# Column sums asked a product later, scaling shared by two engines, and copies and sums near the changes of pair in another order

## What is computed

```python
# attention over chunks of 32 queries, with 16 keys to the left, 8 to the right and 8 memory keys
x = attn_out.transpose(0, 2, 1, 3).reshape(3072, 512)
# first layer, d_ff = 1536
x = (x @ w_a) * (x @ w_b) @ w_out
# second layer: E = 8 experts, F = 1024, all tokens through all experts
P = exp(logits - logits.max()), logits = x @ w_gate      # 3072 x 8
for _ in range(8):
    P /= P.sum(1, keepdims=True) + 1e-09
    P /= P.sum(0, keepdims=True) + 1e-09
    P *= N / E
for e in range(E):
    h = maximum(x @ w1[e], 0)
    out += P[:, e:e+1] * (h @ w2[e])
```

## Time and profile before

| | |
|---|---|
| runs | 2672.65, 2674.56, 2677.81 us, median 2674.56 |
| profiled execution | 2671.34 us |
| its span | 2669.6 us, 39021 instructions |
| PE busy | 2586.2 us, 97% |
| DVE busy | 1570.4 us, 59% |
| ACT busy | 994.2 us, 37% |
| POOL busy | 1610.1 us, 60% |
| mean granted clock of TensorE | 0.991 of full |

### The profile page before, as it was taken

How to read it: one execution, slowest core, us unless ns; L and a number is a source line. 1 busy time by engine, 2 the same in 40 slices (tenths; PEclk the granted TensorE clock), 3 DMA queues, 4 the chain that set the end, 5 groups by cost and what they waited for, 6 DMA issues and landing times.

```text
span 2669.6 us, 39021 instructions
## 1 busy us (share of the span) xinstructions
PE 2586.2 (97%) x14946; PEld 2128.0 (80%) x14946; DVE 1570.4 (59%) x2295; ACT 994.2 (37%) x1718; POOL 1610.1 (60%) x1304
## 2 busy tenths in 40 slices
PE   7879999999999999999999999999998999999998
PEld 6658878878777888888887888888886888888887
DVE  3464454554558555555566666666667566666665
ACT  4544332232333334433333333333334433333333
POOL 0055510010276777777766777777778777777776
PEclk9999999999999999999999999999999999999999
DMA  7745644334355666666664645454544564545453
GB/s 184 162 156 210 224 178 158 143 142 159 133 208 192 254 247 226 258 256 234 234 257 183 250 183 220 182 206 188 222 180 173 188 246 173 222 182 220 184 219 115
DMA packets 193136, 530.48 MB, mean 199 GB/s; under 512 B 55544, under 2 KB 128184, under 8 KB 173752
## 3 DMA queue, kind: packets, MB, share of 16 engines
q1 hardware_dynamic: 192952, 527.99, 54.2%
HBM read 367.41 MB, written 160.60 MB: 198 GB/s over the span
## 4 chain that ended last, share of the span: by engine, by line
PE 87%; DVE 4%; POOL 3%; issue 2%; DMA 1%; ACT 1%; SPq 1%; ACTq 0%; DVEq 0%; POOLq 0%
PE bank L940 43%; PE bank L1039 21%; PE bank L1017 19%; PE bank L863 2%; POOL X L735 1%; DMA W<-w_kept 1%; POOL H L813 1%; PE bank L902 1%; DVE tmp L1595 1%; PE bank L878 1%; SPq L570 0%; PE bank L890 0%; ACT X L1260 0%; DMA Qr<-in_q_dram 0%; DVE hid L1798 0%
## 5 line engine op out<-in xcount | busy, mean ns | idle before, releaser
L940 PE MATMUL bank<-X,W 128*128 128x512 f32 x5550 | 1403.8, 391 | 22.8 <-ACT tmp L1310 9.6
L940 PEld LDWEIGHTS bank<-X,W 128*128 128x128 f32 x5550 | 1043.5, 189 | 250.9 <-issue 23.6
L813 POOL TENSOR_TENSOR H<-tmp,H 128x512 fp32r<-128x512 f32 x448 | 577.0, 1300 | 295.4 <-ACT H L1435 293.4
L1039 PE MATMUL bank<-H,W2n 128*128 128x512 f32 x2688 | 682.8, 390 | 7.7 <-DVE Y L1648 4.1
L1648 DVE TENSOR_TENSOR Y<-Y,bank 128x512 f32<-128x512 f32 x752 | 497.1, 683 | 265.1 <-PE bank L1039 265.1
L1039 PEld LDWEIGHTS bank<-H,W2n 128*128 128x128 f32 x2688 | 504.2, 188 | 115.6 <-issue 7.0
L1435 ACT ACTIVATE H<-tmp 128x512 fp32r<-128x512 f32 x448 | 276.8, 630 | 475.1 <-DVE tmp L1678 248.3
L1017 PE MATMUL bank<-W,hid 128*128 128x512 f32 x1536 | 388.1, 391 | 1.8 <-DVE Y L1625 1.8
L1017 PEld LDWEIGHTS bank<-W,hid 128*128 128x128 f32 x1536 | 289.2, 189 | 62.5 <-DVE Y L1625 2.2
L735 POOL TENSOR_TENSOR X<-Y,X 128x1024 fp32r<-128x1024 f32 x30 | 79.0, 2638 | 385.2 <-ACT X L1260 385.2
L1625 DVE SCALAR_TENSOR_TENSOR Y<-bank,gate,Y 128x512 f32<-128x512 f32 x224 | 167.0, 747 | 167.3 <-PE bank L1017 166.2
(11 more groups left out here) (111 smaller groups left out, 2160.6 us busy)
## 6 DMA issues: line engine op xcount, KB each, us to landing
W<-w_kept SPq DMA_DIRECT2D x88, 1792.0 KB, 11.1
W2n<-w2n_kept SPq DMA_DIRECT2D x64, 1536.0 KB, 8.2
w_kept<-W SPq DMA_DIRECT2D x44, 1792.0 KB, 8.1
raw<-in_moe_w_dram SPq DMA_DIRECT2D x64, 512.0 KB, 4.4
w2n_kept<-W SPq DMA_DIRECT2D x32, 1024.0 KB, 7.9
w2n_kept<-tmp SPq DMA_DIRECT2D x64, 512.0 KB, 8.0
W2n<-w2n_kept SPq DMA_DIRECT2D x64, 256.0 KB, 3.0
W<-w_kept SPq DMA_DIRECT2D x12, 1024.0 KB, 9.1
```

The costliest lines, as they stand in the source:

```text
L813: nc.gpsimd.tensor_tensor(H[:, pos, 1], hidden_at(k, pos), H[:, pos, 0].bitcast(F32), ALU.subtract).then_inc(h_lo, 1)
L940: last = nc.tensor.matmul(into[:, :], W1[:, c % 2, ws, w_slot, kc, :], X[:, pos, xs, kc, :], start=(start and kc == 0 and n == 0), stop=(k ...
L1039: last = nc.tensor.matmul(b_half[pair][half][:, :], W2n[k % 2][:, a, blk, half * P:(half + 1) * P], H[:, h, b, :], start=(q in (0, 5) and ...
```

## The change

Four things are changed.

1. `TOTALS`: the totals asked behind the products of position 6 are now asked behind those of position 0 of the next step.
2. `scale_first`: DVE scales four of the eight tiles, ACT the other four in step 5; the last scaling of the gates signals a semaphore of its own, and the accumulation into an ACT tile waits for ACT.
3. At the changes of pair: one x sum (`operand_sum 4`) moves from the end of a step into the next one, a gated product ahead of an x sum and of adds, POOL's low part of w2's sums ahead of three x pieces, a store on SP behind the loads of step 32, and the copy of x piece 6 behind copy_u.
4. On ACT, at u = 0 the pieces 2 and 3 of `up_hi` move behind copy_v; in all steps from 32 on, `hidden_hi(k, 0)` moves behind copy_v.

```diff
@@ -260,7 +260,9 @@
         g_total = sem("g_total")
         g_chain = sem("g_chain")
+        g_fin = sem("g_fin")
         g_scaled = sem("g_scaled")
+        g_scaled2 = sem("g_scaled2")
         s_out = sem("s_out")
@@ -330,6 +332,10 @@
         U_AT = (tmp[:, 4, :], tmp[:, 5, :])
         V_N, B11_T1, B12_T3, T2_AT = (tmp[:, i, :] for i in range(4))
+
+
+        def y_tile(n):
+            return Y[:, n // 2, n % 2 * TB:(n % 2 + 1) * TB]
         def hidden_at(k, pos):
@@ -646,7 +652,8 @@
                 keep_down(M1 + u)
                 keep_t_hi(u)
-                keep_t_lo(u)
+                if u + 1 < V2:
+                    keep_t_lo(u)
                 if u == 8:
                     store_gates()
@@ -655,6 +662,8 @@
                     load_gates(u)
                 fetch_blocks(u)
+                if u == V2:
+                    keep_t_lo(V2 - 1)
                 if u == V2 + 3:
                     store(0)
@@ -787,10 +796,10 @@
             block_sums(V2 - 1)
             down_lo(M1 + V2 - 1)
-            for i in range(1, 4):
+            operand_lo(4, 1, 1)
+            block_sums_lo(V2 - 1)
+            for i in range(2, len(X_POOL)):
                 operand_lo(4, 1, i)
-            block_sums_lo(V2 - 1)
-            operand_lo(4, 1, 4)
@@ -833,9 +842,9 @@
                     operand_lo(first_use(w + 2), p, 0)
                 hidden_lo(k, 5)
+                hidden_lo(k, 6)
                 if n is not None:
                     operand_lo(n, p, 4)
-                hidden_lo(k, 6)
         @block.tensor
@@ -931,7 +940,7 @@
-            TOTALS = [(u, pos) for u in range(2, 6) for pos in (1, 3, 6)][1:1 + SINKHORN]
+            TOTALS = [(u, pos) for u in range(2, 6) for pos in (0, 1, 3)][2:2 + SINKHORN]
             def product(c, pos, into, start):
@@ -1042,7 +1051,7 @@
             def transpose_gates():
-                pe.wait_ge(g_scaled, NG)
+                pe.wait_ge(g_fin, 1)
                 n = N // P // 2
                 for i in range(2):
@@ -1295,10 +1304,10 @@
-            def operands_late(w):
+            def operands_late(w, late=(5, 6)):
                 n = first_use(w)
                 if n is not None:
-                    for pos in (5, 6):
+                    for pos in late:
                         operand_hi(n, unit_of(w)[0], pos, last_chain(w - 1))
@@ -1378,17 +1387,26 @@
                 if u + 1 < V2:
                     up_hi(c + 1, (0, 1))
+                if u == UE + 1:
+
+                    act.wait_ge(g_fin, 1)
+                    act.wait_ge(y_acc, NG * (M1 + UE))
+                    for t in range(SUB):
+                        nc.scalar.activation(y_tile(t), y_tile(t), ACT.Copy,
+                                             scale=gate[:, t, 0:1]).then_inc(g_scaled2, 1)
                 if u == 0:
                     act.wait_ge(f_lo, 4 * M1)
...
                     act.wait_ge(e_lo, 4 * u)
                 copy_u(c, u_at)
-                if u + 1 < V2:
+                if 0 < u < V2 - 1:
                     up_hi(c + 1, (2, 3))
                 down_hi(w)
...
                 first_h_hi(u, 0, bank[BANK_A][:, :], 0, 0)
                 copy_v(c, v_at)
+                if u == 0:
+                    up_hi(c + 1, (2, 3))
                 if n is not None:
                     operand_hi(n, p + 1, 1, c)
@@ -1455,7 +1473,7 @@
                 if (u, 1) in OUT_SLOTS:
                     copy_out(1, OUT_SLOTS.index((u, 1)), b_gate)
-                operands_late(w)
+                operands_late(w, (5,))
                 if n is not None:
                     operand_hi(n, p, 0, c)
@@ -1468,9 +1486,7 @@
                 if k > 0:
                     hidden_hi(k - 1, 6)
-                hidden_hi(k, 0)
-                if n is not None:
-                    operand_hi(n, p, 1, c)
+                operands_late(w, (6,))
                 if k == 0:
@@ -1479,6 +1495,9 @@
                     act.wait_ge(h_lo, NP * (k - 1) + H_LO.index(1) + 1)
                 copy_v(c, V_N)
+                hidden_hi(k, 0)
+                if n is not None:
+                    operand_hi(n, p, 1, c)
                 if (u, 4) in OUT_SLOTS:
                     copy_out(1, OUT_SLOTS.index((u, 4)), b_gate)
@@ -1613,6 +1632,8 @@
                     gated = p > 0 or e > 0
                     by = gate[:, p * NG + n, e:e + 1]
+                if w == M1 + UE and g == NG // 2:
+                    dve.wait_ge(g_scaled2, SUB)
                 if i == 0 and g == 0:
@@ -1720,8 +1741,13 @@
                 link(nc.vector.tensor_scalar(col_t, b_sum[:, 0:E], EPS, float(E) / N, ALU.add, ALU.mult))
                 link(nc.vector.reciprocal(col_t, col_t))
-                link(nc.vector.tensor_tensor(by_expert, by_expert,
-                                             col_t.unsqueeze(2).to_broadcast([P, E, N // P]), ALU.mult))
+                scaled = nc.vector.tensor_tensor(by_expert, by_expert,
+                                                 col_t.unsqueeze(2).to_broadcast([P, E, N // P]), ALU.mult)
+                if i < SINKHORN - 1:
+                    link(scaled)
+                else:
+                    scaled.then_inc(g_fin, 1)
+                    dve.wait_ge(g_fin, 1)
             def sinkhorn_slot(n):
@@ -1732,10 +1758,10 @@
                 dve.wait_ge(y_acc, NG * (M1 + UE))
-                for n in range(NG):
-                    y = Y[:, n // 2, n % 2 * TB:(n % 2 + 1) * TB]
-                    nc.vector.tensor_scalar(y, y, gate[:, n, 0:1], None, ALU.mult).then_inc(g_scaled, 1)
-                dve.wait_ge(g_scaled, NG)
+                for n in range(SUB, NG):
+                    nc.vector.tensor_scalar(y_tile(n), y_tile(n), gate[:, n, 0:1], None,
+                                            ALU.mult).then_inc(g_scaled, 1)
+                dve.wait_ge(g_scaled, NG - SUB)
             def g_lo(v, n, f, l):
@@ -1838,8 +1864,6 @@
                 dve.wait_ge(c_21, c + 1)
                 first_h_lo(u, 3, u_at, 1, 0)
-                if n is not None:
-                    operand_sum(n, p + 1, 4)
                 if u == 1:
                     shift_logits()
@@ -1853,10 +1877,11 @@
                     accumulate(w - 1, 0)
                     accumulate(w - 1, 1)
+                    operand_sum(first_use(w), p - 1, 4)
+                    accumulate(w - 1, 2)
                     operand_lo(first_use(w), p - 1, 5)
-                    accumulate(w - 1, 2)
+                    gated(u, 0)
                     accumulate(w - 1, 3)
-                    gated(u, 0)
                     accumulate(w - 1, 4)
                     sum_22(c, V_N, V_N)
@@ -1869,15 +1894,17 @@
                 if k > 1:
                     add_blocks(u - 2, 6)
+                add_blocks(u - 1, 1)
+                if first_use(w) is not None:
+                    operand_sum(first_use(w), p - 1, 4)
+                if n is not None:
+                    operand_sum(n, p, 1)
+                add_blocks(u - 1, 2)
                 if first_use(w) is not None:
                     operand_lo(first_use(w), p - 1, 5)
-                add_blocks(u - 1, 1)
-                if n is not None:
-                    operand_sum(n, p, 1)
-                add_blocks(u - 1, 2)
+                gated(u, 0)
                 if n is not None:
                     operand_sum(n, p, 3)
-                gated(u, 0)
                 add_blocks(u - 1, 3)
                 sum_22(c, V_N, V_N)
@@ -1890,7 +1917,6 @@
                 if n is not None:
                     operand_lo(n, p, 3)
-                    operand_sum(n, p, 4)
             add_blocks(M2 - 2, 6)
             for q in range(1, NP):
```

More of the change, by code:

```diff
@@ L1871, in _ @@
                     add_blocks(u - 2, 6)
+                add_blocks(u - 1, 1)
                 if first_use(w) is not None:
-                    operand_lo(first_use(w), p - 1, 5)
-                add_blocks(u - 1, 1)
+                    operand_sum(first_use(w), p - 1, 4)
                 if n is not None:
@@ L1877, in _ @@
                 add_blocks(u - 1, 2)
+                if first_use(w) is not None:
+                    operand_lo(first_use(w), p - 1, 5)
+                gated(u, 0)
                 if n is not None:
                     operand_sum(n, p, 3)
-                gated(u, 0)
                 add_blocks(u - 1, 3)
```

## The result

The changed kernel took 2690.57 us (median of 5 runs, 2684.14 to 2693.31) against 2673.77 (5 runs, 2670.11 to 2677.81): ratio 1.0062, 95% interval 1.005 to 1.0073. It is slower, by 16.8 us. The forecast was 2684, its own range 2677 to 2693. The profiled execution took 2684.14 us, 12.8 more than the one of before.

What follows compares the result with a forecast made beforehand. TensorE (PE) was taken to set the time, busy all 19.04 us of a step. From 2671.3 us, gains of 20.5 and a repeating cost of 30.1 gave 2680.9, plus 3.2 for the median: 2684 us, range 2677 to 2693.

Steps and rivals of the forecast that it cites:

- repeating part: Steps of the last phase: hidden_hi behind copy_v lets POOL block DVE's second gated product; 0.51 us per step, 30.1 us lost.
- entry: Entry to the second layer (u = 0): copy_v freed from up_hi pieces waiting for POOL; 7.0 us gained, least 4.
- column sums: Three PE waits for a round's last reduction, 9.2 us with slow clock, leave 4.7; gain 4.5 us, bounds 2 and 6.5.
- first change: First change of pair (u = 31 to 33): three PE waits, 7.36 us lost; gain 7.0, bounds 5 and 7.4.
- second change: Second change of pair (u = 63 to 65): copy_v moves ahead but DVE is late; gain 2 us, bounds 0 and 5.
- gains together: Entry, column sums and both changes of pair together: 20.5 us gained, from 14 to 24.
- sum: Whole kernel: 2671.3 - 20.5 + 30.1 = 2680.9, with 3.2 for the median 2684.1 us, 0.35% slower.
- third rival: Gains fall short: over 5 us wait with slow clock at second change, entry wait returns; gains 10, 2694 us; chance 0.08.
- the four steps with output: Steps 65 to 68, where PE also transposes outputs: some 0.35 us more room, so 4 x 0.16 us lost.
- the tail: End of the kernel, where PE waits for POOL's chain anyway: 0.4 us of the repeating cost.
- The POOL instruction that was feared: Column sums: a POOL instruction falling on DVE's two-input L1798 might block it, making PE's wait 1.8 us instead of 1.2.
- three obstacles: First change of pair: x sum before an accumulation, first hidden copy before copy_v, t_lo store before weights' DMA; 7.0 us gain.

Runs made afterwards that it cites:

- kernel 1: The changed kernel with hidden_hi(k, 0) ahead of copy_v again in all 64 steps, everything else kept; 2662.94 us, ratio 0.9956 to the kernel before.
- kernel 2: The kernel before with one line moved: hidden_hi(k, 0) behind copy_v in all 64 steps; 2701.09 us, ratio 1.0099 to the kernel before.
- kernel 3: The changed kernel, orders kept, but POOL starts hidden_lo(k, 0) only after DVE's gated product 1 has ended; 2665.83 us, ratio 0.9965 to the kernel before.
- kernel 5: The kernel before with the entry edit alone: at u = 0 pieces 2 and 3 of up_hi behind copy_v; 2668.83 us, ratio 0.9976.
- kernel 8: Changed kernel, hidden_hi(k, 0) behind copy_v at k = 0 only, POOL reordered at u = 0, eighth accumulation ahead of gated product 3 at k = 0; 2662.65 us.
- kernel 9: Changed kernel, hidden_hi(k, 0) behind copy_v at k = 0 only, plus the eighth accumulation ahead of gated product 3 at k = 0; 2661.79 us.
- kernels 1 to 4: kernel 1, kernel 2, kernel 3 and a fourth: the changed kernel with hidden_hi(k, 0) behind copy_v at k = 0 only, 2662.74 us.
- kernel 7: The kernel before with the scaling and the edits at the changes of pair, hidden_hi(k, 0) ahead of copy_v; 2668.69 us, ratio 0.9977.

## Why the prediction was right, and where its sizes were off

| term | forecast | measured |
|---|---|---|
| repeating part | +30.1 | +27.6 (kernel 1), +26.0 (kernel 2) |
| entry | -7.0 | -4.2 in the trace; alone -5.6 |
| column sums | -4.5 | -4.5 in the trace (copy_u of 2 to that of 6); alone -3.9 |
| first change | -7.0 | -4.4 (24 to 34, kernel 1) |
| second change | -2 | -0.7 (52 to 76, kernel 1) |
| gains together | -20.5 | -12.2 |
| sum | +9.6 | +16.8 |

(-12.2 and +27.6 make 15.4; the 1.4 to 16.8 lie within the scatter of the two sets of runs.)

The direction and its cause came as forecast. The size did not come from one term: the gains were taken 8.3 us too large and the cost 2.5 too large, and the second error covers a part of the first. With gains of 12.2 the outcome is nearer to the third rival (gains of 10, 2694) than to the 2684 of the sum, though not by all of its reasons.

**The repeating part.** The mechanism is shown, from both sides (kernels 1 and 2) and by taking only the overlap away (kernel 3). Lags were forecast as 0.50, 0.71 and 0.22 and are 0.50, 0.70 and 0.23; the product's mean 1.6, and is 1.587; the wait 0.26 in some 60 cases, and is 0.24 in nearly all of 62; the step 19.5, and is 19.54. The rule of the Trainium skill that stood beside the price (SBUF — State Buffer, "Who interferes with whom": the first of the two blocks the other fully) agrees with the 1.60: the product ends 0.55 behind POOL's end, so most of its 0.69 of work lies behind it. The term was 2.5 us too large. A step costs 0.49 instead of 0.51, which makes 57 x 0.49 = 27.9 instead of 29.1; the four steps with output cost 0.1 together instead of 0.6, the tail 0.9 instead of 0.4; the rest lies within the scatter.

**The entry.** 7.0 was taken and 4 named as the least; 4.2 came (7.1 lost before, 2.9 after). The step that failed: "The pieces are then needed only by u = 1's weights, and POOL's share of those does not move." It does not move, and that is the trouble: it was hidden behind the copy_v wait, and is what PE waits for next. The wait itself shrank by only 1.2 us, from 3.92 to 2.72; the other 3.0 are the lower clock that followed it in before and did not follow it in after. In kernel 3 it did, and there the step gained 1.2 us in all, so two thirds of this term hang on something that differs from one execution to the next.

**The column sums.** Two waits of 1.33 against 1.2 to 1.8 forecast, accumulations 0.30 late against 0.35. (The first total moved three groups back, as the order ahead of the prediction shows; "Asked two groups later" is a slip that no sum uses.) The POOL instruction that was feared did not block L1824 (0.69 in both cases), but another blocked the multiplication of the round, which also reads two tiles in SBUF. DVE and POOL of after in the first of the two rounds, and the multiplication of the next, undisturbed:

```profile
796.73 2.14 POOL L707 TENSOR_TENSOR W<-raw,W 128x512 fp32r<-128x512 f32 x2 [2.03 <-ACT W L1240]
797.37 1.08 DVE L1744 TENSOR_TENSOR gate<-gate,lg 128x192 f32<-128x192 f32 x1
...
801.84 0.54 DVE L1744 TENSOR_TENSOR gate<-gate,lg 128x192 f32<-128x192 f32 x1
```

The second round has the same (820.68, 1.04). So some 0.5 us of each 1.33 is the collision of the earlier trace rows again, in a place that was not walked, and the match with the 1.2 of the sum, which has no such term, is in part luck. The 4.5 contains 3.4 us for two stretches at the lower clock; kernel 5 shows that an execution of the old code can be without them.

**The first change.** The failed step is "The change moves each of the three obstacles", from which 7.0 was taken; the 4.4 that came is less than the least that was allowed, 5. They are gone, but two waits took their place (0.99 and 1.31 us, 3.2 with what follows them). The second came from the accumulation standing behind the gated product, since kernel 8 and kernel 9 take it away; 1.1 of its 1.31 is what the collision of the earlier trace rows adds to the product (1.80 less 0.69). The first has the same look: an x sum (L1572) starting at 1390.03 inside a POOL instruction (1388.91, 2.85 us), and lasting 2.82 us; that one was not tried. I had walked DVE against POOL in the step that repeats, and not in this one.

**The second change.** The gain of 2 did not come: of the 0.7 in the table 0.6 is the DMA wait at step 71 (1.19 in before, 0.64 in kernel 1), and the two steps from 63 to 65 take 50.1 us in before and 50.0 in kernel 1. DVE was late in its own right, as said, and most came back in one wait of 4.9 us with a stretch at the lower clock: the part of the third rival that did occur. The windows of after, behind that wait:

```profile
2025.00:2030.00 5.00, 5.00 (x12) 3.94 (x13) 4.96 (x5) 2.75 (x4) 4.92 (x4) 0.50 0.31 84
```

DVE's lateness contains here a gated product of 2.36 us, blocked by a POOL instruction of 2.41.

**The level.** The profiled execution of after is 6.4 us below its median. Its first copy_u of the first layer stands at 178.0 us, in before at 180.1, in the profiles of kernels 1 to 4 at 180.1 to 185.5, with code that is the same up to there. That shows a scatter of this size ahead of everything that was changed. Whether it accounts for the 6.4 stays open, as the other executions have no trace.

## What to carry to other kernels

When a line moves in a loop, price it per pass before the places it was moved for, and set each engine's new start beside that of the engine that can block it: here 0.23 us of lead, some 60 times over, outweighed every wait that was removed. When a wait is removed, ask which result arrives next at the same place; three of four gains here were capped by the one that stood behind. A collision costs only by what queues behind the blocked instruction. In two places here (kernels 3 and 9) it was enough to let the urgent instruction go first, though the collision itself stayed.

## What was not expected of the hardware

- The fall of the clock behind a wait is not certain. Behind PE waits of 1.8 us, with the same code, windows show 0.66 in two executions (before and kernel 7) and 1.00 in another (kernel 5). Behind the entry's wait of 2.7 it was 1.00 in six executions and 0.50 in one. Behind the waits of 1.33 in after no such stretch was seen (1.00 in both windows of 5 us).
- A blocked DVE instruction takes its turn back: in after, POOL's three low parts that start beside the end of the blocked product at k = 0 took 4.24 us, where three take 3.78 in the earlier trace rows. Nearly all of that is in the first of them, 1.72 instead of 1.29.
- POOL needs almost no lead: 0.05 us (1413.33 to 1413.38) made a product of 0.69 take 1.80.
